# Sink values stacked in pieces, first weight splits and loads moved, fewer filler matmuls, one q/k split a slot later

## The reference

```python
scores = scale * np.matmul(q, k.transpose(0, 1, 3, 2))
keep = (pos[None, :] < n_sink) | ((rel >= 0) & (rel < window))     # 4 sink keys, window of 128
scores = np.where(keep, scores, -1000000000.0)
a = np.exp(scores - np.max(scores, axis=-1, keepdims=True))
a = a / (np.sum(a, axis=-1, keepdims=True) + 1e-09)
x = np.matmul(a, v)                          # tokens x 512
h = x @ w1_in;  x = np.maximum(0.01 * h, h) @ w1_out
h = x @ w2_in;  x = (h / (1 + np.exp(-h))) @ w2_out
```

## Time and profile before

| | |
|---|---|
| median of three executions | 673.38 us (671.8 to 674.53) |
| the profiled execution | 672.19 us, span 669.8 us |
| PE / DVE / ACT / POOL busy over the span | 96% / 42% / 45% / 18% |
| mean granted TensorE clock | 0.989 of full |
| TensorE's first score matmul | 13.57 us |
| TensorE's `hidden(0)` | 68.67 us |

### The profile page before, as it was taken

How to read it: one execution, slowest core, us unless ns; L and a number is a source line. 1 busy time by engine, 2 the same in 40 slices (tenths; PEclk the granted TensorE clock), 3 DMA queues, 4 the chain that set the end, 5 groups by cost and what they waited for, 6 DMA issues and landing times.

```text
span 669.8 us, 9081 instructions
## 1 busy us (share of the span) xinstructions
PE 642.4 (96%) x3113; PEld 528.3 (79%) x3113; DVE 278.2 (42%) x646; ACT 299.9 (45%) x676; POOL 119.1 (18%) x165
## 2 busy tenths in 40 slices
PE   5989899989989999999999999999999999999997
PEld 3667688877768888887888888888888888888886
DVE  3669555555535555552222225333322222212222
ACT  3778556565536556642333335333322333223332
POOL 4767333242314233310000000000000000000000
PEclk8899999999989999999999999999999999999999
DMA  4664234334331223111011122233211111201101
GB/s 114 174 191 118 81 114 119 111 96 126 97 94 33 79 65 112 32 60 35 1 63 64 64 63 95 94 98 103 103 75 31 64 63 64 95 0 64 64 0 63
DMA packets 16940, 53.27 MB, mean 80 GB/s; under 512 B 2560, under 2 KB 2560, under 8 KB 16896
## 3 DMA queue, kind: packets, MB, share of 16 engines
q1 hardware_dynamic: 16512, 52.63, 25.9%
q10 hardware_dynamic: 384, 0.07, 0.1%
HBM read 49.55 MB, written 3.15 MB: 79 GB/s over the span
## 4 chain that ended last, share of the span: by engine, by line
PE 78%; issue 7%; DVE 5%; ACT 3%; POOL 2%; DMA 2%; POOLq 0%; SPq 0%; ACTq 0%; DVEq 0%
PE h_ps L797 36%; PE y_ps L823 33%; PE o_ps L763 3%; DMA qk_raw<-qk 2%; PE t_ps L731 2%; PE s_ps L718 1%; DVE wout L600 1%; DVE win L594 1%; ACT wout L456 1%; PE y_ps L707 1%; ACT prob L413 1%; DVE g L605 1%; DVE pT L551 1%; POOL k_hl L333 1%; PE t_ps L741 1%
## 5 line engine op out<-in xcount | busy, mean ns | idle before, releaser
L797 PE MATMUL h_ps<-x,win 128*128 128x512 f32 x1152 | 284.6, 394 | 9.1 <-DVE win L594 5.3
L797 PEld LDWEIGHTS h_ps<-x,win 128*128 128x128 f32 x1152 | 214.0, 189 | 54.2 <-DVE win L594 6.9
L463 ACT ACTIVATE g_f<-h_ps 128x512 f32<-128x512 f32 x96 | 57.4, 598 | 268.9 <-PE h_ps L797 268.7
L823 PE MATMUL y_ps<-g,wout 128*128 128x512 f32 x576 | 146.5, 395 | 1.2 <-PE o_ps L763 1.2
L823 PE MATMUL y_ps<-wout,g 128*128 128x512 f32 x576 | 138.2, 389 | 0.0
L600 DVE TENSOR_TENSOR wout<-w_raw,wout 128x512 fp32r<-128x512 f32 x64 | 47.2, 737 | 192.9 <-ACT wout L456 192.9
L823 PEld LDWEIGHTS y_ps<-wout,g 128*128 128x128 f32 x576 | 108.1, 188 | 22.4
L823 PEld LDWEIGHTS y_ps<-g,wout 128*128 128x128 f32 x576 | 103.9, 188 | 20.7 <-issue 1.9
L605 DVE TENSOR_TENSOR g<-g_f,g 128x512 fp32r<-128x512 f32 x96 | 66.0, 687 | 99.9 <-ACT g L465 99.9
L413 ACT ACTIVATE prob<-sm,neg_max 128x260 f32<-128x260 f32 (+1 forms) x96 | 47.0, 490 | 56.5 <-DVE neg_max L543 56.4
L465 ACT ACTIVATE g<-h_ps 128x512 fp32r<-128x512 f32 x96 | 56.9, 593 | 0.0
(11 more groups left out here) (76 smaller groups left out, 415.4 us busy)
## 6 DMA issues: line engine op xcount, KB each, us to landing
w_raw<-w SPq DMA_DIRECT2D x64, 512.0 KB, 3.3
qk_raw<-qk SPq DMA_DIRECT2D x48, 260.0 KB, 4.5
v_raw<-vt SPq DMA_DIRECT2D x12, 256.0 KB, 4.4
y<-qk_raw SPq DMA_DIRECT2D x12, 256.0 KB, 2.3
vs_raw<-vsink ACTq DMA_DIRECT2D x8, 8.0 KB, 4.5
```

The source lines that it names most:

```text
L463: nc.scalar.activation(g_f32[:, F % 2, :], h_ps[:, :], func, alpha=slope)
L797: ins = mm(h_ps[:, :], win[:, split_slot[split_of[F]], wp, c * P:(c + 1) * P], x[:, xp, c, tokens(F)], start=(c == 0 and wp == HI and xp = ...
L823: ins = mm(y_ps[d][:, :], a[:, d * P:(d + 1) * P], r, start=(first and wp == HI and gp == HI), stop=(last and wp == LO))
```

## The change

- `stack_sink_values` is cut into seven pieces: the cast, the reduction, the copy, one subtraction each, one multiplication each. Piece i is issued on VectorE in slot 3 + i, behind `invert_sums` and ahead of `take_half` and `scale_half`. Nothing of it is left ahead of the k splits of tile 0.
- SyncE's first four weight loads stand at slots 9, 11, 13 and 15 of its program instead of 4 to 7.
- The first splits: win 0 in slot 14 (was 17), wout 0 in slot 16 (was 18), win 1 in slot 17 (was 18). wout 1 stays in slot 19, and from win 2 on all is as before. SyncE's load of weight 4 moves with wout 0, from slot 18 to 16.
- Half 0 of q, k of tile 5 (the sixth) is split in slot 19 instead of 18, on ScalarE ahead of `take_hidden(0)`.
- In slots 8 to 18 TensorE issues one filler matmul instead of three.

```diff
--- before.py
+++ after.py
@@ -67,6 +67,7 @@
 
 
     FS = PAIRS * TB + 3
+    first_loads = (9, 11, 13, 15)
     LAST = NPAIR + 4
 
 
@@ -75,7 +76,9 @@
     for j, s in enumerate(first_step):
         was, was_out = at, at_out
         start, i = s - s % FT, s % FT
-        if s < FT:
+        if s < 2:
+            at, at_out = 3 * s - 5, 3 * s - 3
+        elif s < FT:
             at, at_out = s - 2, s - 1
         elif i < FT - KEPT:
             at = at_out = s - 6
@@ -220,7 +223,7 @@
             return sum(has_sinks(s // 2) for s in range(e))
 
         def j_split(T):
-            return 1 if T < TB else 2
+            return 1 if T < TB else 3 if T == TB else 2
 
         split_1 = {(T, 3): T + 1 for T in range(TB)}
         split_1.update({(T, 0): T for T in range(TB + 1, TILES)})
@@ -274,8 +277,8 @@
                     if j == 2:
                         load_qk(T + 1, 1)
                         load_v(T + 1)
-                if PAIRS <= a < 2 * PAIRS:
-                    load_w(a - PAIRS)
+                if a in first_loads:
+                    load_w(first_loads.index(a))
                 load_ws(a - FS)
             for F in range(LAST - FS, NSTEP):
                 load_ws(F)
@@ -501,8 +504,8 @@
                 if (T, j) in split_1:
                     high_qk(split_1[T, j], 1)
                 if a == FS:
+                    high_qk(T + 1, 0)
                     take_hidden(0)
-                if a == FS:
                     exp(2 * a + 1)
                     take_hidden(1)
                 elif not head:
@@ -516,8 +519,8 @@
                     high_win(s)
                 if not head:
                     evacuate(F, 0)
-                    if j == j_split(T) and T + 1 < TILES:
-                        high_qk(T + 1, 0)
+                if a > FS and j == j_split(T) and T + 1 < TILES:
+                    high_qk(T + 1, 0)
             for F in range(LAST - FS, NSTEP):
                 evacuate(F - 1, 1)
                 if F + 1 < NSTEP:
@@ -620,25 +623,29 @@
                         wait(dve, out_stored[d], 16 * b)
                         nc.vector.tensor_copy(out_sb[:, d, :], y_ps[d][:, :]).then_inc(out_dve, 1)
 
-            def stack_sink_values():
-
-
-                dve.wait_ge(vs_loaded, 16 * B * REP)
-                dve.wait_ge(const_step, CONSTS)
-                nc.vector.tensor_copy(vs_hi[:, :, :], vs_raw[:, :, :]).then_inc(vs_step, 1)
-                dve.wait_ge(vs_step, 1)
-                nc.vector.tensor_reduce(block_of[:, :],
-                                        ident[:, :].rearrange("p (r h s) -> p h r s", r=REP, h=H),
-                                        mybir.AxisListType.XY, ALU.add).then_inc(vs_step, 1)
+            def stack_sink_values(piece):
+
+
                 n = H * NS
-                nc.vector.tensor_copy(vs_part[:, :, :], vs_hi[:, :, :].bitcast(F32)).then_inc(vs_step, 1)
-                dve.wait_ge(vs_step, 3)
-                for r in (1, 3):
-                    rows = slice(r * n, (r + 1) * n)
+                if piece == 0:
+                    dve.wait_ge(vs_loaded, 16 * B * REP)
+                    nc.vector.tensor_copy(vs_hi[:, :, :], vs_raw[:, :, :]).then_inc(vs_step, 1)
+                elif piece == 1:
+                    dve.wait_ge(const_step, CONSTS)
+                    nc.vector.tensor_reduce(block_of[:, :],
+                                            ident[:, :].rearrange("p (r h s) -> p h r s", r=REP, h=H),
+                                            mybir.AxisListType.XY, ALU.add).then_inc(vs_step, 1)
+                elif piece == 2:
+                    dve.wait_ge(vs_step, 1)
+                    nc.vector.tensor_copy(vs_part[:, :, :], vs_hi[:, :, :].bitcast(F32)).then_inc(vs_step, 1)
+                elif piece < 5:
+                    dve.wait_ge(vs_step, 3)
+                    rows = slice((2 * piece - 5) * n, (2 * piece - 4) * n)
                     nc.vector.tensor_tensor(vs_part[rows, :, :], vs_raw[rows, :, :],
                                             vs_hi[rows, :, :].bitcast(F32), ALU.subtract).then_inc(vs_step, 1)
-                dve.wait_ge(vs_step, 5)
-                for b in range(B):
+                else:
+                    b = piece - 5
+                    dve.wait_ge(vs_step, 5)
                     nc.vector.tensor_tensor(vs_st[:, b, :, :],
                                             vs_part[:, b, :].unsqueeze(1).to_broadcast([P, H, D]),
                                             block_of[:, :].unsqueeze(2).to_broadcast([P, H, D]),
@@ -647,7 +654,6 @@
             nc.vector.memset(filler[:, :], 0.0).then_inc(filler_ready, 1)
             nc.vector.memset(row_sum[:, :, :, 1:2], 1e-9).then_inc(norm_step, 1)
             nc.vector.memset(prob_sink[:, :, :, :, :], 0.0).then_inc(zeroed, 1)
-            stack_sink_values()
             for half in range(2):
                 dve.wait_ge(k_high, half + 1)
                 h0, h1 = half * (H // 2), (half + 1) * (H // 2)
@@ -664,6 +670,8 @@
                     low_pair(a - 2)
                 if a in inverted_in:
                     invert_sums(inverted_in[a])
+                if 3 <= a < 3 + 5 + B:
+                    stack_sink_values(a - 3)
                 if not head and a < NPAIR:
                     mask_max(2 * a)
                 if a in turned_in:
@@ -840,7 +848,7 @@
                         weigh_values(a - 2)
                     if a in turned_in and has_sinks(turned_in[a] // 2):
                         weigh_sinks(turned_in[a])
-                    fill(3)
+                    fill(3 if a < 2 * PAIRS else 1)
                     continue
                 if a == FS:
                     scores(2 * a)
```

## The result

The kernel after took 668.03 us (median of 7 runs, 666.72 to 669.0), the kernel before 671.8 us beside it (7 runs, 670.98 to 674.53): a ratio of 0.9934, with 0.9918 to 0.9949 as its 95% interval. The forecast was 668.8 us and a range of 664.3 to 672.6. It is faster by 3.8 us where the sum said 4.6; the forecast started from 673.38 us, and before measured 1.6 us less in these runs, so the two differences partly cancel in the absolute number.

What follows compares the result with a forecast made beforehand. The prediction took the mutual waits of ScalarE and VectorE, 5.27 us a pair of slots, as the bound, not TensorE. Its terms, -4.6 - 3.4 + 2.4 + 2.6 - 1.6 = -4.6, took 673.38 to 668.8 us, range 664.3 to 672.6.

Steps and rivals of the forecast that it cites:

- The ring of ScalarE and VectorE: Each pair of slots: ScalarE and VectorE wait on each other, closing in 5.27 us without TensorE, which fillers pad.
- The start: Tile 1's first q, k load issues at 8.9 instead of 13.54, and the rest moves with it: -4.6 us.
- The pieces: Slots 6 and 8: stacking pieces ahead of scale_half wait for GpSimd, +2.4 us; +0.95 if free.
- The first splits: Slots 14 and 16: early weight splits put ScalarE's and VectorE's parts in sequence ahead of the masks, +1.3 each, +2.6 us.
- The load of slot 7: Slot 7: without two weight loads ahead, the q/k half is no longer late, -3.4 us over slots 6 to 10.
- The late load of slot 13: Slot 13: q/k half lands 9 us after v's issue, ScalarE stands 2.7 us, 671.5 us; rival, chance 0.10.
- Slots 18 and 19: Between hidden(0) and hidden(1): moving weight and q, k splits out of slot 18 closes TensorE's gaps, -1.6 us.
- The fillers: Slots 8 to 18: two fewer a slot take 0.44 us off TensorE and none off the period: 0.
- The clock at the start: Slots 3 to 5: TensorE's clock falls and is still low there, +2.5 us, 671.3 us; rival, chance 0.10.
- The clock in slots 8 to 18: With fillers gone the clock falls: +3.5 us per pair at half clock, 683 us with four; rival, chance 0.05.

Runs made afterwards that it cites:

- the last three kernels: Changed kernel, pieces out of slots 6 and 8, weight splits in 17 and 18, weight loads at 9, 13, 15, 17; three, one, no fillers: 663.22, 661.1, 662.42 us.
- e4_splits_back: The changed kernel with win 0 split in slot 17 and wout 0, win 1 in slot 18 again: 664.99 us, 0.9876 of before.
- e2_loads_only: The kernel before with only the first four weight loads moved to slots 9, 11, 13, 15: 671.05 us, 0.9974 of before.
- e1_stack_only: The kernel before with only the sink-value stacking cut into pieces and moved to slots 3 to 9: 667.54 us, 0.991 of before.
- e10_loads_early: The changed kernel with the first four weight loads at slots 4 to 7 again: 668.49 us, 0.9959 of before.
- e5_pieces_moved: The changed kernel with both subtractions in slot 7, the multiplications in slots 9 and 19, none in 6 and 8: 665.56 us, 0.9918 of before.
- e3_fill3: The changed kernel with three fillers in every slot again: 668.52 us, 0.9938 of before.
- e6_qk_slot18: The changed kernel with half 0 of tile 5's q, k split in slot 18 again: 667.8 us, 0.9947 of before.
- e11_both_order: The changed kernel with pieces out of slots 6 and 8, weight splits in slots 17 and 18, weight loads at 9, 13, 15, 17: 661.1 us, 0.9843 of before.

## Why the prediction was right, and where it was not

**The ring of ScalarE and VectorE** was the bound, as forecast. Pairs of slots without a late load or an extra instruction (10 to 12 and 14 to 16 in the last three kernels) take 5.25 to 5.32 us with three, one and no fillers a slot, and TensorE's real work is 86% of the time with none. The rest of its 99% was padding.

**The start** was right to 0.1 us: 8.86 against 8.9 for the load, 24.60 against 24.5 for slot 6. The load went behind k's first subtraction, and that had GpSimd's q subtraction beside it, as forecast.

**The pieces** were right at the blocked price: 2.22 us measured by moving them, 2.4 forecast; the multiplication of slot 8 took 1.47 us (forecast 1.3). By the rule of the Trainium skill, page "SBUF — State Buffer", section "Who interferes with whom", a VectorE instruction with two SBUF inputs contends with a GpSimd one that reads SBUF, and a reduction never does. The trace agrees, with the 0.94 and 1.47 us above, and with the reduction of slot 4, which ran beside GpSimd's subtraction and took no longer than the 0.28 us of before:
```profile
19.76 1.32 POOL L336 TENSOR_TENSOR k_hl<-qk_raw,k_hl 128x528 fp32r<-128x528 f32 x1
...
20.78 0.26 DVE L635 TENSOR_REDUCE block_of<-ident 128x8 f32<-128x128 f32 x1
```
It takes 0.26 us and ends ahead of GpSimd's instruction, at 21.04 against 21.08.

**The first splits** cost 2.96 us (e4_splits_back), 2.6 forecast. The step was right: ScalarE's and VectorE's part do come one after the other. The term was a little small: the pairs of slots grew by 1.40 and 1.56 us instead of 1.3 each, 0.07 of it because VectorE's part in slot 16 took 0.76 us where I had 0.69 from the earlier trace rows.

**The load of slot 7** was right in size and cause for the kernel before, and not for the change as a whole. Moving the weight loads alone took 3.42 us off slots 6 to 10 (e2_loads_only), where the term had 3.4. But the prediction gave all of it to the weight loads, and the other parts take most of the same wait away. e1_stack_only lost the wait of slot 7 with the weight loads in place, and with start and pieces moved the move of the loads is worth 0.7 to 1.0 us. Of the 2.79 us of before, 0.9 go because the piece in slot 6 makes ScalarE ask later. The load behind two weight loads was also quicker: 10.15 us in the earlier trace rows was one landing time, and the same place in the queue gave 8.1 us in e1_stack_only and 9.2 in e10_loads_early. The sum came out because the wait goes once, whichever part removes it; had one added the parts' separate gains, it would have been counted twice.

**The late load of slot 13** is the rival that came in part: 0.26 us in the kernel after, 1.88 and 2.05 in the two kernels with three fillers and the loads in the same order. I had 0, with 0 to 2 as its bounds. The +0.43 for slots 10 to 14 is mostly it. That it was small here may be luck: the prediction had no ground to tell 0.3 from 2.

**Slots 18 and 19**: -1.63 against -1.6. One move would have been enough: that of the weight splits, which costs 3 us ahead of `hidden(0)`, and that of the q, k split each close the gap alone. The forecast had one price and one gain for them and did not ask whether the gain could be had for less.

**The fillers**: 0, as forecast. **The clock at the start** fell in part (0.75 between 15 and 20 us), and cost nothing, since slot 6 came to within 0.1 us. **The clock in slots 8 to 18** stayed full in the kernel after. The rival did come for a few microseconds in two kernels with the same fillers and the same early splits, e5_pieces_moved and e10_loads_early, at 0.6 to 0.7 us. So the kernel after was lucky there too. In the kernels with the splits back it was full in the one profile of each, with and without fillers.

What remains open is what decides how soon a q/k half lands behind a weight load (the instruction load beside the two slow ones is a rival to chance), and why the clock fell behind the pause of an early split in two kernels and not in the others that have them (after, e3_fill3, e6_qk_slot18).

## What to carry to other kernels

A high busy share proves nothing where fillers pad an engine: compare the period of the steps with what each engine's real work needs, and test it by taking the fillers out. Before a step is moved to an earlier stage, ask whether one of the things that share its place can be moved at no cost instead; here moving the q, k split alone bought what two early weight splits bought for 3 us. Put small VectorE instructions with two SBUF inputs where GpSimd is idle and no engine waits for what follows: the same pieces cost 2.2 us less a slot further on. By their durations, (0.94 - 0.29) + (1.47 - 0.68) = 1.4 us of that was GpSimd's doing, and the rest their place in the ring. When two parts of a change remove the same wait, count it once. And don't price a load by one landing time; look for how much it varies in the same place.

## What the runs showed of the hardware

The end of one stretch differs between executions with nothing in the program to explain it. Near 190 us TensorE waits 2.64 us for GpSimd's x in each of these kernels. Its next 12 matmuls, at that place, in the kernel before, in e2_loads_only and in e11_both_order:
```profile
194.08 4.58 PE L797 MATMUL h_ps<-x,win 128*128 128x512 f32 x12 [2.64 <-POOL x L312]
```
```profile
192.96 3.02 PE L804 MATMUL h_ps<-x,win 128*128 128x512 f32 x12 [2.64 <-POOL x L315]
```
```profile
184.67 5.46 PE L807 MATMUL h_ps<-x,win 128*128 128x512 f32 x12 [2.64 <-POOL x L315]
```
4.58, 3.02 and 5.46 us for the same work behind the same wait. In the 12 us around it the granted clock was 0.86, 1.00 and 0.73: the half clock (1.2 GHz) was there for a short stretch, for none, and for a longer one. From `hidden(1)` to the end of the span they took 594.4, 592.8 and 595.7 us. All thirteen profiles sort this way: 592.7 to 592.8 us where the 12 matmuls took 3.0 us (four kernels), 594.1 to 594.4 where they took 4.3 to 4.6 (eight), 595.7 in the one with 5.46.

The same was seen in slots 15 and 16: behind an equal wait of 1.78 us the granted clock was 0.50 for 3 us in e5_pieces_moved and stayed 1.00 in the kernel after.

Two q/k halves issued at the same times to 0.01 us, in the same order, were there 1.86 us apart (7.15 and 5.29 us, e3_fill3 and after).

VectorE's and GpSimd's subtractions held each other up, whichever started second: VectorE's 1.21 us and GpSimd's 0.74 with GpSimd ahead by 0.07 us (e10_loads_early), 0.76 and 1.17 with VectorE ahead by 0.17 (after).
